# Routing by a running sum, the last product of layer 1 in two halves, and a later weight load in a three-stage kernel

## The chip, the cores and the metric

The kernel runs on one core of a Trainium2 chip. Its time is the device time of one execution in microseconds (us). Here it is a chain of dependent stages with one stream of instructions for each engine: TensorE (PE, with its weight loads as PEld), VectorE (DVE), ScalarE (ACT), GpSimd (POOL) and SyncE (SP, which here only issues DMAs). The streams meet through semaphores: an instruction waits until a semaphore has reached a value, and raises one when it is done.

## What is computed

Three layers follow each other: an attention with the queries pooled in pairs, a mixture of experts with a capacity (layer 1), and a second mixture of experts with a skip test and a residual (layer 2). All is float32. There are 2 x 8 heads over 1152 keys and 576 pooled queries, hence 1152 tokens of width 512; 8 experts with a hidden width of 1024.

```python
# attention (B=2, H=8, S=1152, D=64), pooled queries
q_pool = q.reshape(B, H, S // 2, 2, D).mean(axis=3)
scores = scale * np.matmul(q_pool, k.transpose(0, 1, 3, 2))
attn = softmax(scores)                 # sum + 1e-9
x = (attn @ v) -> [1152 tokens, 512]

# layer 1: a token goes to its best expert if that has room (capacity 288)
logits = x @ w_gate
expert_idx = np.argmax(logits, axis=1)
for i in range(N):                     # in the order of tokens
    if counts[e] < capacity:
        pos[i] = counts[e]; counts[e] += 1; keep[i] = True
h = relu(disp @ w1[e]); y = h @ w2[e]
out[i] = gate_w[i] * y                 # 0 where not kept

# layer 2: only tokens with x @ w_skip > 0
logits = xc @ w_gate2; e_idx = argmax(logits)
y[mask] = gate_w[mask] * (relu(xc[mask] @ w1[e]) @ w2[e])
out[do_compute] = xc + y               # else out = x
```

## The kernel before, in words

**Attention.** One head after the other. TensorE makes scores, turns the exponentials over with transposes, multiplies them by V and turns the result back (`turn_back`, L768, of the output tile `OT` that VectorE copies from the matmul buffers in `copy_output`, L1194). VectorE divides by the sums (`output_logits`, `output_x`), SP stores each head's 64 columns in DRAM (`store_x`, L436, four DMAs a head) and the logits of the routing come out of the same product, added over heads by `add_logits` (L1240) and `add_last_logits`.

**Routing** runs twice, as `for m in range(2)` on every engine (L855 on TensorE, L1362 on VectorE): m = 0 for layer 1, over 9 tiles of 128 tokens, and m = 1 for layer 2, over 14 tiles of 128 slots. VectorE finds each token's expert (`r_hot`, one column in eight is 1). TensorE counts with matmuls by triangular and full matrices of ones (L871 to L882) how many tokens of the same expert stand ahead of each one, and the total of each expert. These counts are in PSUM when `pos_ready` is raised. VectorE then makes of the totals how many grains of 64 rows each expert takes (`r_cmp`, `r_nt`), where each expert's grains begin (`r_sq`, `r_base`), adds that to the counts (`r_pos`), and cuts the slot into a tile number and a row in the tile (`r_which`, `r_inside`; L1404 to L1434). From these come `r_tile` and, three tiles at a time, `r_place`; POOL multiplies `r_tile` by token numbers (L655), and TensorE adds up in L890 which token stands in which slot. VectorE turns that into the list `rows_in` (L1443), and POOL fetches the first 128 rows from DRAM with an indirect DMA (`load_x`, L606) into `xraw`. Meanwhile VectorE prepares the gates (`r_gcut`, `r_ids`), TensorE sorts them (L898), and VectorE writes the tables of tiles and experts (`tab_n`, `tab_done`, `tab_grain`; `tables_ready` after L1464). Nearly every one of these VectorE instructions waits for the one before through a semaphore (`link`, L1328).

**Fillers.** Where TensorE would idle, it runs products of the identity with itself whose result nobody reads (`keep_busy`, L835, and the shorter `keep_briefly`). Their number is written into the program: 11 before the counting, 18 (m = 0) or 19 (m = 1) behind it, 16 or 12 behind the sorting of the gates. TensorE works its stream off in order, so what stands behind fillers starts only when they are through. The profile shows two records for each filler.

**Experts.** A tile of 128 rows is two grains of 64, which may belong to two experts. Weights lie in rings of four matrices (`w1ring`) and three (`w2ring`), loaded by SP in 4 pieces (`load_matrix`, L385). The upper grain's matrix is copied into `wright` by VectorE or ScalarE (`fill_right`, L323). A step on TensorE is `hidden_product(t)`, `y_product(t - 1)`, `turn_x(t + 1)`, `turn_hidden(t)`. Layer 1 has 10 tiles with these inputs and layer 2 has 9; the loops are written for the largest number, and an `If` in the body leaves the unused rounds empty. In layer 1, VectorE also makes the logits of layer 2 for each finished tile (`next_logits`, L1350: 9 multiply-and-add passes over `ysb`), after copying it. For the last tile this isn't done by VectorE: ScalarE copies the product (`ylast`, L1163), TensorE turns it (`turn_y`), ScalarE copies that (`yT`), TensorE multiplies by the weights of the logits, and ScalarE copies the nine columns into `logits2` (L1167). VectorE waits for that with `lg_copied`, for a value that it loads from the table `tab_n` (L1386), then starts the routing of layer 2.

**SP's order around the end of attention** is: store the last head (four DMAs, L458), wait until all is stored, load the first `w2` matrix of layer 1 (L464), wait until the first tile's rows have arrived, load the second `w2` matrix, and so on up to `wnext`, the weights for `next_logits`.

## Time and profile before

| | |
|---|---|
| median of 3 runs | 618.69 us (618.34 to 618.9) |
| the profiled execution | 618.62 us, of which the span of the profile is 616.9 us |
| granted TensorE clock, mean over the span | 0.995 of full speed |
| PE busy | 594.9 us, 96% of the span |
| DVE, ACT, POOL busy | 315.1, 266.9, 191.5 us |
| chain of waits | PE 90%, DMA 2%, DVE 2%, ACT 2%, "issue" 2% |

The chain of waits is followed back from the last instruction, at each step to what released it. TensorE's busy time holds the fillers too, so a busy TensorE isn't always one that does work. The three layers meet at two places: from about 270 to 291 us (attention to layer 1) and from about 446 to 467 us (layer 1 to layer 2). "Span" is what the trace covers; the time of the execution is 1.7 us more.

### The profile page before, as it was taken

The numbers are of one execution on the slowest core, as the hardware profiler recorded it, in microseconds if no ns is written. First come the engines' busy times: TensorE is split into PE (matmuls) and PEld (weight loads), VectorE is DVE, ScalarE is ACT, GpSimd is POOL, SyncE is SP. The second block draws the span as 40 slices with busy tenths as digits, with TensorE's granted clock in tenths as the row PEclk, the third lists the DMA queues.
The fourth block names the chain that finished last, engine by engine and source line by source line (L and its number), as shares of the span: only waits on it lengthen the run. The fifth ranks groups of instructions, "written<-read, shape, count | busy, mean of one in ns | idle before, by whom it ended". The sixth has DMA issues, their size and how long they took to land.

```text
span 616.9 us, 12447 instructions
## 1 busy us (share of the span) xinstructions
PE 594.9 (96%) x3719; PEld 352.3 (57%) x3720; DVE 315.1 (51%) x666; ACT 266.9 (43%) x439; POOL 191.5 (31%) x168
## 2 busy tenths in 40 slices
PE   8899999999999999998999999999999999999993
PEld 7677787877777777777333333333395333333331
DVE  5457565657575756656355652965574220322220
ACT  4655565655565656520244444444102444444410
POOL 4785635344453800001012221122211122222222
PEclk9999999999999999999999999999999999999997
DMA  8979818171721062006999397780846798841111
GB/s 201 291 184 258 186 39 173 39 166 45 153 50 26 11 232 87 22 9 208 399 391 409 124 352 275 284 307 29 305 174 229 274 312 322 321 150 43 45 52 61
DMA packets 42637, 111.61 MB, mean 181 GB/s; under 512 B 16020, under 2 KB 16020, under 8 KB 41536
## 3 DMA queue, kind: packets, MB, share of 16 engines
q1 hardware_dynamic: 38528, 99.03, 50.5%
q0 software_dynamic: 4080, 12.22, 5.7%
q8 instruction: 15, 0.25, 0.2%
q14 instruction: 14, 0.11, 0.1%
HBM read 102.68 MB, written 12.06 MB: 186 GB/s over the span
## 4 chain that ended last, share of the span: by engine, by line
PE 90%; DMA 2%; DVE 2%; issue 2%; ACT 2%; POOLq 0%; POOL 0%; SPq 0%; DVEq 0%; ACTq 0%
PE psum L929 41%; PE psum L704 14%; PE psum L718 11%; PE psum L752 9%; PE psum L916 4%; PE psum L838 3%; PE psum L780 3%; PE psum L764 1%; PE psum L748 1%; DMA xraw<-moe_in,rows_in 1%; DVE probs L1181 1%; ACT probs L1019 1%; PE psum L931 1%; DMA qraw<-in_q_dram 1%; DMA res<-moe_in,idx_r 1%
## 5 line engine op out<-in xcount | busy, mean ns | idle before, releaser
L929 PE MATMUL psum<-w1ring,XT 128*64 x304 | 134.5, 595 | 0.8 <-ACT XT L1126 0.4
L929 PE MATMUL psum<-w2ring,HT 128*64 x304 | 133.7, 592 | 1.7 <-DVE wright L323 1.7
L931 PE MATMUL psum<-wright,XT 128*64 128x512 f32 x304 | 134.5, 595 | 0.0
L931 PE MATMUL psum<-wright,HT 128*64 128x512 f32 x304 | 133.7, 592 | 0.0
L1181 DVE TENSOR_SCALAR_CACHE_REDUCE probs<-psum 128x1152 f32<-128x1152 f32 x72 | 97.5, 1357 | 62.6 <-PE psum L704 62.6
L1019 ACT ACTIVATE probs<-probs,nmax 128x1152 f32<-128x1152 f32 x72 | 90.7, 1260 | 45.6 <-DVE probs L1181 45.6
L704 PE MATMUL psum<-KT,QT 128*128 128x384 f32 x480 | 102.0, 350 | 3.0 <-DVE probs L1181 1.7
L929 PEld LDWEIGHTS psum<-w2ring,HT 128*64 128x64 f32 x304 | 41.5, 137 | 87.3 <-issue 87.3
L704 PEld LDWEIGHTS psum<-KT,QT 128*128 128x128 f32 x480 | 80.2, 188 | 15.0 <-issue 7.9
L929 PEld LDWEIGHTS psum<-w1ring,XT 128*64 128x64 f32 x304 | 40.1, 137 | 79.8 <-issue 79.8
L718 PE MATMUL psum<-ident,probs 128*128 128x128 f32 x648 | 82.0, 275 | 1.1 <-ACT probs L1019 0.6
L718 PEld LDWEIGHTS psum<-ident,probs 128*128 128x128 f32 x648 | 72.7, 140 | 9.2 <-issue 3.7
L1133 ACT ACTIVATE hid<-psum,slot_gate 128x1024 f32<-128x1024 f32 x19 | 21.2, 1114 | 125.2 <-PE psum L931 125.2
L1026 ACT COPY PT<-psum 128x512 f32<-128x512 f32 x88 | 48.4, 588 | 60.3 <-PE psum L718 60.3
L752 PE MATMUL psum<-PT,V 128*64 128x512 f32 x256 | 62.2, 605 | 0.0
L323 ACT COPY wright<-w1ring 128x1024 f32 x60 | 58.1, 1040 | 0.0
L323 DVE COPY wright<-w2ring 128x1024 f32 x76 | 49.1, 700 | 14.3 <-DMA w2ring<-in_moe_w_dram 14.2
L1348 DVE TENSOR_TENSOR orow<-psum,res 128x512 f32<-128x512 f32 x9 | 6.2, 691 | 97.0 <-PE psum L931 88.1
L1355 DVE CUSTOM_DVE_ANT_0 psum<-ysb,wnext 128x512 f32<-128x512 f32 x81 | 52.9, 723 | 0.0
L595 POOL COPY idx_x<-rows_in 128x1 int32 x15 | 8.8, 585 | 142.0 <-PE psum L916 142.0
L335 POOL CAST KT<-kraw 128x2304 fp32r<-128x2304 f32 x7 | 14.7, 2106 | 87.3 <-PE psum L704 82.8
L931 PEld LDWEIGHTS psum<-wright,HT 128*64 128x64 f32 x304 | 41.5, 137 | 0.0
(169 smaller groups left out, 645.7 us busy)
## 6 DMA issues: line engine op xcount, KB each, us to landing
w1ring<-in_moe_w_dram SPq DMA_DIRECT2D x64, 512.0 KB, 6.9
w2ring<-in_moe_w_dram SPq DMA_DIRECT2D x64, 512.0 KB, 7.1
qraw<-in_q_dram SPq DMA_DIRECT2D x30, 288.0 KB, 10.0
kraw<-in_k_dram SPq DMA_DIRECT2D x14, 576.0 KB, 9.2
V<-in_v_dram SPq DMA_DIRECT2D x8, 576.0 KB, 4.0
moe_in<-zero SPq DMA_DIRECT2D x9, 256.0 KB, 3.1
wnext<-in_next_w_dram SPq DMA_DIRECT2D x1, 2304.0 KB, 17.1
out_dram<-moe_in SPq DMA_DIRECT2D x1, 2304.0 KB, 9.4
```

Source lines behind the costliest of these rows:

```text
L323: copy(wright[k][:, part * PIECE:(part + 1) * PIECE], piece_of(k, slot, part).rearrange("p o f -> p (o f)")).then_inc(filled, 1)
L704: mm = pe.matmul(dst, QT[par][:, piece, q0:q0 + P], KT[par][:, b * S + c * KB:b * S + (c + 1) * KB], start=(i == 0), stop=(i == 2 * len(pa ...
L718: mm = pe.transpose(bank(T_BANK + place % 3)[:, i * P:(i + 1) * P], src, ident[:])
L752: mm = pe.matmul(psum[rows, PV_BANK, :], V[par][:, b * KT_N + j, :], PT[:, j, :], start=(j < 2), stop=False, skip_group_check=True)
L916: return pe.matmul(place[:, chunk * P:(chunk + 1) * P], src, ident[:], is_transpose=True, start=first, stop=False, skip_group_check=True)
L929: pe.matmul(psum[0:GRAIN, b, :], lhs[:, c * P:c * P + GRAIN], left, start=first, stop=last, skip_group_check=True)
L931: return pe.matmul(psum[GRAIN:P, b, :], lhs[:, c * P + GRAIN:(c + 1) * P], wright[k][:, cols], start=first, stop=last, skip_group_check=True)
L1019: nc.scalar.activation(probs[:, t, :], probs[:, t, :], ACT.Exp, bias=nmax[:, t:t + 1], scale=-1.0, accum_out=den[:, t:t + 1]).then_inc(pro ...
L1026: nc.scalar.copy(dst, bank(T_BANK + place % 3, cols)).then_inc(turned_by_act, 1)
L1133: nc.scalar.activation(hid[:].rearrange("p (c f) -> p c f", c=2), psum[:, HID_BANK:HID_BANK + 2, :], ACT.Relu, scale=g).then_inc(relu_read ...
L1181: nc.vector.tensor_scalar(probs[:, t, :].rearrange("p (c k) -> p c k", c=3), scores_in(h, t), -SCALE, None, ALU.mult, ALU.min, accum_out=n ...
L1355: nc.vector.tensor_tensor_reduce(out=bank(JUNK_BANK + e % 2), in0=ysb[:], in1=wnext[:, e, :], scale=1.0, scalar=0.0, op0=ALU.mult, op1=ALU ...
```

## The change

Six things are changed.

1. **Running sum (VectorE, both routings).** The totals are clamped (`r_held`), and one scan over 8 elements makes of them the running sum of rounded grains (`ends`). Adding a large number (`ROUND`) makes each partial sum round to a multiple of 64; a matmul of `whole` by `half_grain` adds the half grain that this needs. That replaces comparing, summing, multiplying by `earlier` and summing; and later, for the tables, multiplying by `upto` and summing. Some steps are joined into `scalar_tensor_tensor`, and some waits between neighbours fall away, since a semaphore of their own is waited for later.
2. **Fillers.** 14 instead of 18 and 19 behind the counting, 8 instead of 16 and 12 behind the sorting of the gates.
3. **SP.** The first `w2` matrix of layer 1 is loaded only when the first tile's rows have arrived. Of the last head's four stores, three no longer wait for the second batch's rows.
4. **The end of attention.** The last `OT` is copied in two halves of 256 columns, and `add_logits` goes ahead of that copy.
5. **The last product of layer 1** (`last_y_product`) is made in two halves of 256 columns into two banks. ScalarE copies the first while the second is made. The turned tile (`yT`) and the nine logits are now copied by VectorE.
6. **Gates of layer 1** are finished (`sum_gates`) before `rows_in` instead of behind it.

```diff
@@ SP
-            store_x(H - 1)
+            last_rows = token_rows(x_dram[0])
+            for i, written in ((0, 2 * H - 1), (1, 2 * H - 1), (3, 2 * H - 1), (2, 2 * H)):
+                sp.wait_ge(x_written, written)
+                parts, tiles, rows = last_rows[i]
+                sp.dma_start(rows[:, :, (H - 1) * D:H * D], xpair[parts, tiles, :]).then_inc(x_stored, 16)
             attention_over(sp)
             sp.wait_ge(zeroed, NT * 16)
             sp.wait_ge(x_stored, 16 * 4 * H)
+            sp.wait_ge(x_loaded_[0], 16)
             load_matrix(SECOND, 0, 0)
-            sp.wait_ge(x_loaded_[0], 16)
             load_matrix(SECOND, 0, 1)
@@ TensorE
                 pe.matmul(place_of(0, n), before[:], hot, start=True, stop=False, skip_group_check=True)
+                pe.matmul(place_of(n, n + 1), whole[:], half_grain[:].unsqueeze(1), start=False, stop=False, skip_group_check=True)
...
-                keep_busy((18, 19)[m], HID_BANK + 1)
+                keep_busy((14, 14)[m], HID_BANK + 1)
...
-                keep_busy((16, 12)[m], HID_BANK + 1)
+                keep_busy((8, 8)[m], HID_BANK + 1)
...
+                def last_y_product(t):
...
+                    for half in range(2):
+                        for c in range(FC):
...
+                            at = c * DM + half * 2 * P
+                            mm = product(SECOND, HT, (Y_BANK, X_BANK)[half], c, slice(at, at + 2 * P), slot,
+                                         c == 0, c == FC - 1, 2 * P)
+                        mm.then_inc((y_half, y_done)[half], 1)
@@ ScalarE
+                    act.wait_ge(y_half, 1)
+                    nc.scalar.copy(ylast[:, 0:2 * P], bank(Y_BANK, 2 * P)).then_inc(ylast_copied, 1)
                     act.wait_ge(y_done_[0], rest + (2 + START))
-                    nc.scalar.copy(ylast[:], bank(Y_BANK)).then_inc(y_copied_[0], 1)
-                    act.wait_ge(y_turned, 1)
-                    nc.scalar.copy(yT[:], bank(YT_BANK)).then_inc(yt_ready, 1)
-                    act.wait_ge(lg_done, 1)
-                    nc.scalar.copy(logits2[:, bass.ds(rest + 1, 1), :].rearrange("p o c -> p (o c)"), bank(LG_BANK, E + 1)
-                                   ).then_inc(lg_copied, 1)
+                    nc.scalar.copy(ylast[:, 2 * P:4 * P], bank(X_BANK, 2 * P)).then_inc(ylast_copied, 1)
@@ VectorE
+                link(nc.vector.tensor_scalar(r_held[:], tot, float(cap if m == 0 else B * SQ) + half, 1.0 + half, ALU.min, ALU.max))
+                link(nc.vector.tensor_tensor_scan(ends[:, 1:E + 1], r_held[:], r_held[:], ROUND + P, ALU.add, ALU.max))
...
                 with dve.Fori(1, NSLOT - 1) as t:
                     with dve.If(t < rest + 1):
                         step(t)
-                if m == 1:
+                if m == 0:
+                    for i in range(2):
+                        half = slice(i * 2 * P, (i + 1) * 2 * P)
+                        dve.wait_ge(y_turned, i + 1)
+                        nc.vector.tensor_copy(yT[:, half], bank(YT_BANK + i)[:, half]).then_inc(yt_ready, 1)
+                    at = bass.ds(rest + 1, 1)
+                    dve.wait_ge(lg_done, 1)
+                    nc.vector.tensor_copy(logits2[:, at, :].rearrange("p o c -> p (o c)"), bank(LG_BANK, E + 1)
+                                          ).then_inc(lg_copied, 1)
+                else:
                     copy_y(m, rest + 1)
```

VectorE's stream in the routing of layer 1, from the counts to `r_tile`, before:

```order
L1335 TENSOR_TENSOR r_cmp<-psum,grain_steps 128x8x5 [waits pos_ready]
L1338 TENSOR_REDUCE r_nt<-r_cmp 128x8 [waits route_step]
L1335 TENSOR_TENSOR r_sq<-r_nt,earlier 128x64 [waits route_step]
L1338 TENSOR_REDUCE r_base<-r_sq 128x8 [waits route_step]
L1420 TENSOR_SCALAR r_over<-psum 128x72 [waits route_step]
L1335 TENSOR_TENSOR r_pos<-psum,r_base 128x72 [waits route_step]
L1335 TENSOR_TENSOR r_pos<-r_pos,r_over 128x72 [waits route_step]
L1335 TENSOR_TENSOR r_pos<-r_pos,r_hot 128x72 [waits route_step]
L1338 TENSOR_REDUCE r_whole<-r_pos 128x9 [waits route_step]
L1431 TENSOR_SCALAR r_inside<-r_whole 128x9 [waits route_step]
L1432 TENSOR_SCALAR r_which<-r_whole 128x9 [waits route_step]
L1433 TENSOR_TENSOR r_tile<-iota_slot,r_which 128x126 [waits route_step]
```

The same stretch of VectorE's stream in the changed kernel (the row on `ends` is the scan):

```order
L1438 TENSOR_SCALAR r_held<-psum 128x8 [waits pos_ready]
L1439 SCALAR_TENSOR_TENSOR ends<-r_held 128x8 [waits route_step]
L1445 SCALAR_TENSOR_TENSOR r_kept<-psum,r_hot 128x72 [waits route_step]
L1446 SCALAR_TENSOR_TENSOR r_pos<-ends,psum 128x72
L1363 TENSOR_TENSOR r_pos<-r_pos,r_kept 128x72 [waits kept_ready,route_step]
L1366 TENSOR_REDUCE r_whole<-r_pos 128x9 [waits route_step]
L1452 TENSOR_SCALAR r_inside<-r_whole 128x9 [waits route_step]
L1453 TENSOR_SCALAR r_which<-r_whole 128x9
L1454 TENSOR_TENSOR r_tile<-iota_slot,r_which 128x126 [waits route_step]
```

Eleven instructions stood ahead of `r_tile`, each behind a wait for its neighbour; now there are eight, and two of them have no wait.

VectorE's stream from the last tile's logits in the loop of layer 1 to the start of the second routing, before:

```order
L1358 REGISTER_ALU
L1360 ISA [waits lrow_ready]
L1360 COPY logits<-lrow 128x9
L1497 UNCONDITIONAL_BRANCH
L1496 REGISTER_ALU
L1496 COMPARE_AND_BRANCH
L1386 TENSOR_LOAD tab_n
L1386 ISA x2
L1386 REGISTER_ALU
L1387 TENSOR_SCALAR active<-logits 128x14 [waits lg_copied]
```

And in the changed kernel:

```order
L1388 ISA [waits lrow_ready]
L1388 COPY logits<-lrow 128x9
L1518 UNCONDITIONAL_BRANCH
L1517 REGISTER_ALU
L1517 COMPARE_AND_BRANCH
L1524 COPY yT<-psum 128x256 [waits y_turned] x2
L1527 ISA [waits lg_done]
L1527 COPY logits<-psum 128x9
L1414 TENSOR_LOAD tab_n
L1414 ISA x2
L1414 REGISTER_ALU
L1415 TENSOR_SCALAR active<-logits 128x14 [waits lg_copied]
```

Three copies now stand between the end of the loop and the load of `tab_n`, and that load stands behind the copy of the last logits.

SP's stream at the end of attention, before and then changed; `moe_in<-xpair` are the stores of the last head, and the first `w2ring` row is the first `w2` matrix of layer 1:

```order
L441 DMA moe_in<-xpair 128x4x64 [waits x_written]
L441 DMA moe_in<-xpair 64x64
L441 DMA moe_in<-xpair 128x4x64
L441 DMA moe_in<-xpair 64x64
L397 DMA w2ring<-in_moe_w_dram 128x1024 [waits zeroed,x_stored,kq_cut,turned_back,logit_step]
L397 DMA w2ring<-in_moe_w_dram 128x1024 x3
L397 DMA w2ring<-in_moe_w_dram 128x1024 [waits x_loaded_0,w2_loaded_0]
```

```order
L457 DMA moe_in<-xpair 128x4x64 [waits x_written]
L457 DMA moe_in<-xpair 64x64 [waits x_written] x2
L457 DMA moe_in<-xpair 128x4x64 [waits x_written]
L392 DMA w2ring<-in_moe_w_dram 128x1024 [waits x_stored,zeroed,x_loaded_0,kq_cut,turned_back,logit_step]
L392 DMA w2ring<-in_moe_w_dram 128x1024 x3
L392 DMA w2ring<-in_moe_w_dram 128x1024 [waits w2_loaded_0]
```

The wait for `x_loaded_0`, the first tile's rows, has moved ahead of the first matrix.

## Rows read from the trace of the kernel before

**Rows 1.** The page, chain that ended last: share of the span by engine.
```profile
PE 90%; DMA 2%; DVE 2%; issue 2%; ACT 2%; POOLq 0%; POOL 0%; SPq 0%; DVEq 0%; ACTq 0%
```

**Rows 2.** Chain of waits, attention to layer 1: start us, us, what.
```profile
271.13 0.46 PE psum L748 x4
...
271.61 0.70 DVE OT L1200
...
276.41 4.12 PE psum L838 x36
...
281.85 0.18 DVE rows_in L1443
...
283.05 6.28 DMA xraw<-moe_in,rows_in
...
290.93 0.64 PE psum L929
```

**Rows 3.** Timeline, first routing: start us, us, engine, line, what [idle before <-releaser].
```profile
276.45 0.20 DVE L1335 TENSOR_TENSOR r_cmp<-psum,grain_steps 128x40 f32<-128x40 f32 x1 [0.51 <-PE psum L867]
...
279.17 0.29 DVE L1433 TENSOR_TENSOR r_tile<-iota_slot,r_which 128x126 f32<-128x126 f32 x1
...
279.64 0.55 POOL L655 TENSOR_TENSOR r_ids<-r_tile,token_id 128x126 fp32r<-128x126 f32 x1 [63.78 <-DVE r_tile L1433]
...
287.20 2.50 DVE L323 COPY wright<-w1ring 128x1024 f32 x4 [1.37 <-issue]
```

**Rows 4.** Timeline of SP's DMA issues at the end of attention.
```profile
280.61 10.58 SPq L397 DMA_DIRECT2D w2ring<-in_moe_w_dram  x8
```

**Rows 5.** Stretches: us, PE, PEld, DVE, ACT, POOL busy, PEclk, DMA share, GB/s.
```profile
286.00:287.00 1.00, 1.00 (x12) 1.00 (x11) 0.00 (x0) 0.00 (x0) 0.00 (x0) 1.00 0.96 340
462.00:463.00 1.00, 1.00 (x11) 1.00 (x11) 0.90 (x4) 0.00 (x0) 0.00 (x0) 1.00 0.44 139
```

**Rows 6.** Line L606 (fetch of rows), second routing, 455 to 470 us.
```profile
DMA to landing us min/median/max: 3.5/5.3/7.2
```

**Rows 7.** Timeline, end of layer 1.
```profile
446.59 0.17 DVE L1360 COPY logits<-lrow 128x9 f32 x1
...
447.26 0.66 PE L975 MATMUL psum<-ident,ylast 128*128 128x128 f32 x4
...
447.95 0.59 ACT L1165 COPY yT<-psum 128x512 f32<-128x512 f32 x1 [0.75 <-PE psum L975]
...
448.59 1.06 PE L982 MATMUL psum<-wcat,yT 128*128 128x9 f32 x8 [0.23 <-ACT yT L1165]
```

**Rows 8.** Chain of waits, end of the kernel: POOL's sequencer in empty rounds of its loop.
```profile
602.76 0.05 POOLq L671
...
604.05 0.05 POOLq L671
```

**Rows 9.** Timeline of VectorE: the one step of layer 1 that starts late on its side.
```profile
393.43 0.69 DVE L1345 COPY ysb<-psum 128x512 f32<-128x512 f32 x1 [1.25 <-issue]
```

**Rows 10.** Timeline, second routing.
```profile
449.98 0.17 DVE L1387 TENSOR_SCALAR active<-logits 128x14 f32<-128x14 f32 x1 [3.21 <-ACT logits L1167]
...
453.09 0.31 DVE L1335 TENSOR_TENSOR r_cmp<-psum,grain_steps 128x144 f32<-128x144 f32 x1
...
455.83 0.36 DVE L1433 TENSOR_TENSOR r_tile<-iota_slot,r_which 128x196 f32<-128x196 f32 x1
...
459.55 0.17 DVE L1443 TENSOR_SCALAR rows_in<-psum 128x14 int32<-128x14 f32 x1 [0.81 <-PE psum L890]
```

**Rows 11.** Chain of waits, second routing.
```profile
462.46 2.77 PE psum L838 x24
465.24 0.45 PE psum L916 x4
```

**Rows 12.** Stretches after TensorE's last product (columns as in rows 5).
```profile
607.00:608.00 1.00, 0.07 (x2) 0.00 (x0) 0.00 (x0) 0.00 (x0) 0.30 (x2) 1.00 0.35 49
...
610.00:611.00 1.00, 0.00 (x0) 0.00 (x0) 0.44 (x1) 0.00 (x0) 0.00 (x0) 0.84 0.00 0
```

More of the change, by code:

```diff
@@ L1425, in _ @@
-                if m == 0:
-                    with nc.allow_low_precision(reason="whole numbers far below 2 ** 24"):
-                        reduce(of(r_whole), of(r_pos), ALU.add)
-                else:
-                    reduce(of(r_slot), of(r_pos), ALU.add)
-                    tt(of(r_whole), of(r_slot), r_drop[:], ALU.add)
-                link(nc.vector.tensor_scalar(of(r_inside), of(r_whole), P - 1, None, ALU.bitwise_and))
+                    dve.wait_ge(kept_ready, 1)
+                tt(of(r_pos), of(r_pos), of(kept), ALU.mult)
@@ L1432, in _ @@
+                with nc.allow_low_precision(reason="whole numbers far below 2 ** 24"):
+                    reduce(of(r_whole), of(r_pos), ALU.add)
+                nc.vector.tensor_scalar(of(r_inside), of(r_whole), P - 1, None, ALU.bitwise_and).then_inc(inside_ready, 1)
                 link(nc.vector.tensor_scalar(of(r_which), of(r_whole), 7, None, ALU.logical_shift_right))
```

152 lines of the change are left out of this document (81 added, 71 removed).

## The prediction, made before the changed kernel had run

> **What bounds the kernel now.** I read the chain of waits by engine first: TensorE holds 90% of it, all else is a few per cent [rows 1]. The steps through experts are paced by TensorE's products, and the change leaves these as they are, except the last one of layer 1. So only the two crossings between layers can move the time. The chain, followed in order of time through them, is the second view. In the first crossing it runs through the copy of the output tile, the turning back, fillers, counting, fillers, the search for the rows, and then one long piece: 6.28 us of the DMA that fetches the first rows, before the first product starts at 290.93 [rows 2]. In the second it goes through ScalarE's copies between TensorE's small products [rows 7], VectorE's routing [rows 10], and the fillers in front of the first turning [rows 11]. The timelines of VectorE and SP, the third view, tell who is near behind the chain.
>
> **The sum** is made against the profiled execution, 618.62 us (span 616.9); the median of the runs is 0.07 above it.
>
> *First crossing, output tile and counting.* The full copy takes 0.70 [rows 2]. A copy of half the columns lies between 0.35 and 0.70; I take 0.42, since a copy has a fixed part. The turning back can then start 0.28 earlier, and its second half waits for nothing. The fillers behind it are unchanged in number and shift along; the added small counting matmul costs about 0.03. `add_logits`, moved ahead of the copy, runs while VectorE waits for TensorE's last product with V. **-0.25** (bounds 0 and -0.35).
>
> *First routing.* From `r_cmp` at 276.45 to `r_tile` at 279.17 [rows 3] eleven linked instructions take 2.72, so 0.247 each. Now there are eight, two of them without a wait, for which I take 0.14: 6 x 0.247 + 0.28 = 1.76, a gain of 0.96. The scan is shown by no row; over 8 elements I take it as one of the others, with bounds 0.17 and 0.6. `r_tile` is then 0.96 + 0.25 = 1.2 earlier, POOL's product, started at 279.64 and 0.55 long, ends at 279.0, and TensorE can add up the rows. It must first be through with the fillers: 36 records took 4.12 [rows 2], so 0.229 each filler of two records, four fewer are 0.92, and with the 0.25 they end 1.17 earlier. Both are ready 1.1 to 1.2 earlier than before, so `rows_in` moves from 281.85 [rows 2] to about 280.75. `sum_gates` now stands ahead of it, but ends at about 280.7 while VectorE would wait for TensorE anyway; if that cover is gone it costs up to 0.7. Beyond the 0.25: **-0.85** (bounds -0.2 and -1.0).
>
> *The first fetch.* In the kernel before, SP began to issue the first `w2` matrix at 280.61 [rows 4], 2.4 us ahead of the fetch, and while the fetch ran the DMA engines moved 340 GB/s at a share of 0.96 [rows 5]. The same fetch in the second routing has no matrix beside it (139 GB/s, share 0.44, [rows 5]) and lands in 3.5 us, against 7.2 for the one that follows it among weights [rows 6]. Holding the matrix back until the rows are there should give 3.5 in place of 6.28: **-2.78** (bounds 0 and -2.8). The last head's stores must have landed: only one of four is still issued behind the last rows, before the counts are in, and it has over 4 us until `rows_in`. What is late next? VectorE's copy of the first weights started at 287.20 [rows 3]. It stands behind the tables, which lose the 1.1, the 0.7 of `sum_gates` and two linked instructions (0.5): it starts at 284.9, and its first of four pieces is there at 285.5, before the product at 290.93 - 3.88 = 287.05. TensorE has eight fillers less (1.83) and is free at about 284.8, so it idles 0.7 until the rows land at 285.5. The fetch stays the bound. The first `w2` matrix, now issued at 285.6, needs about 5 us and is wanted after the first hidden product and the copy of the second tile's weights, near 297. Everything behind it on SP moves back about 2 us: the second and third matrices, and `wnext`. I count this as hidden, since the steps through experts are paced by TensorE.
>
> *End of layer 1.* In the kernel before, turning, ScalarE's copy and the product for the logits follow each other and end at 448.59 + 1.06 = 449.65 [rows 7]. With halves that overlap, this alone would end at about 448.9. But the copies of `yT` have gone to VectorE, and there they stand behind the loop over tiles. Its last logits end at 446.59 + 0.17 = 446.76 [rows 7]. The loop has 12 rounds, of which 8 are used: four empty rounds follow. POOL shows what such rounds cost: three in 604.05 - 602.76 = 1.29, so 0.43 each [rows 8]. VectorE is then free at 446.76 + 1.72 = 448.5, where its first half could have begun at about 447.4 (turning from 447.26). Two copies of 0.42, 0.35 apart, end at 449.3; TensorE's second half of the logits ends at 450.0, VectorE has copied the nine columns at 450.2. Then comes the second thing: the load of `tab_n` into a register stood in VectorE's idle time of 3.21 us before [rows 10] and now stands behind that copy. Its price is in rows 9: 1.25 us of idle time for one loop round, such a load and a few register instructions; less 0.43 it is 0.82. `active` starts at about 451.05 instead of 449.98. The Trainium skill puts the floor of a `tensor_load` at about 600 ns (DMA: Bandwidth & Descriptors, Latency and other measured facts); by it alone the sum would be 0.2 us lower, and the row agrees as far as it holds more than the load.
>
> The last product in halves has twice the instructions. The only products of 256 columns in the trace took 0.46 for 4 records [rows 2], so the 64 records of both halves would take up to 7.4 us, about 0.5 more than exact halves, or nothing more where that end is only modelled; I take 0.15. Together **+1.2** (bounds -0.7, if VectorE is free in time and the load hidden, and +2).
>
> *Second routing.* Before the counts, one instruction is shorter, one wait and `r_drop` are gone: VectorE comes 0.4 sooner to the counts. TensorE's counting then nearly binds, so -0.35. From `r_cmp` at 453.09 to `r_tile` at 455.83 [rows 10] ten linked instructions took 2.74. Seven remain, one without a wait, two on 8 elements only: 1.74, so -1.0. Five fillers less (1.14) let TensorE keep up. **-1.35**, `rows_in` then stands 0.15 earlier than before in all. From there two paths lead to the turning of the first rows, which was at 465.24 behind 24 records of fillers, 2.77 us [rows 11]. Four fillers less are -0.92. The fetch starts about 1.0 after `rows_in`, as in the first crossing (283.05 - 281.85 - 0.18, [rows 2]); `rows_in` ends at 459.55 + 0.17 [rows 10] - 0.15, so it starts at 460.5 and lands by 464.1, level with the fillers (464.2). I take **-0.85** (bounds 0 and -0.92).
>
> -0.25 - 0.85 - 2.78 + 1.2 - 1.35 - 0.85 = -4.9. From 618.62 that is 613.7, and with the 0.07 to the median 613.8.
>
> **Rivals.**
>
> *The halved end costs nothing.* For it: four empty rounds on VectorE might be faster than POOL's, and a load might be fetched while the last copy waits. Against it: the same three kinds of instruction make up a round on both engines, and VectorE's own row of 1.25 us [rows 9] fits POOL's. The stage would then stand as before or better, +1.2 gone: 618.7 - 6.1 = 612.6. Beside this, the Trainium skill gives 51 ns for a branch and 108 ns for a compare-and-branch (Advanced Engine Details and Errata, Control Flow Timing): a round of one and two of these would be 0.27 us, against the row's 0.43, and the sum would be 0.65 lower, halfway to this rival.
>
> *The first fetch isn't faster.* It is the first indirect DMA of the program, and if 6.28 us is its own start and not the matrix beside it, the 2.78 are not earned: 616.6. Against it: its landing at 289.3 comes just as the four pieces of the matrix are through.
>
> *Weights come too late.* The matrices after the first, and the second tile's fetch in between, are set back by some 2 us against a TensorE that is 3.9 us ahead. That second fetch took as long as one product lasts (7.2 in rows 6, between products of about 7), so each us more is paid in full. With 1 to 3 us given back: about 615.8.
>
> *Slower.* The fillers keep TensorE busy at the full clock (granted 1.00, 2.4 GHz), and twelve are gone at the first crossing, nine at the second. In the one place where I see the clock fall, the last product had ended at 607.07, the stretch from 607 was at 1.00, and it went to the lower level (1.2 GHz) within the stretch from 610 [rows 12], some 3.6 us after the product. If the first fetch still takes 6.28, TensorE idles from 284.8 to 288.3, 3.5 us, as long as there; then the first hidden product of about 7 us runs at the lower level, up to +7, which with the unearned 2.78 ends at up to 623.7. It decides from a fetch of over 6 us on; with 3.5 us the idle time is 0.7.
>
> **How the numbers follow.** Forecast 0.52 (613.8), halved end free 0.18 (612.6), fetch as slow as ever 0.13 (616.6), weights late 0.12 (615.8), slower 0.05 (620 to 624). The range of 8 in 10 reaches from 612.4, where the end costs nothing, to 616.6, and leaves out the clock and a part of the fetch. What a measurement can tell is about 0.2%, 1.2 us: faster than 617.5 holds in the forecast and nearly all of the next three, 0.92; within it 0.04; slower 0.04.
>
> **What would show it.** `DMA xraw` in the first crossing at 3.5 to 4 us; the first product at 287; VectorE's first copy of `yT` at about 448.5 less the shift, more than 1 us after the first half of the turning, and `active` 0.7 to 0.9 behind the end of the nine logits' copy; the span between the last product of layer 1 and `active` longer by 1 us or so than before; the `r_tile` rows about 1 us nearer to the counts; the clock at 1.00 throughout. It is wrong if the fetch still takes over 5 us, if TensorE waits for weights or rows in the first two tiles, or if `yT` is copied at once when it is turned.

## The result, and the profile after

| | before | changed |
|---|---|---|
| median | 618.69 us (618.34 to 618.9, 5 runs) | 615.66 us (614.51 to 616.29, 5 runs) |
| the profiled execution | 618.62 us, span 616.9 | 616.29 us, span 614.5 |
| granted TensorE clock over the span | 0.995 | 0.992 |

The ratio is 0.995 (95% interval 0.9939 to 0.9961): 3 us faster, in the predicted range (612.4 to 616.6), and 1.9 us slower than the forecast of 613.8. The profiled execution is the slowest of the five; its clock in the second crossing and its tail, below, account for part of that. TensorE's share of the chain (page, as in [rows 1]) has fallen from 90% to 88%:

```profile
PE 88%; DVE 3%; issue 3%; DMA 2%; ACT 2%; POOLq 0%; DVEq 0%; POOL 0%; SPq 0%; ACTq 0%
```

**First crossing.** The chain of waits, attention to layer 1 (start us, us, what; compare [rows 2]):

```profile
271.55 0.43 DVE OT L1224
...
276.11 3.23 PE psum L840 x28
...
280.66 0.18 DVE rows_in L1467
...
281.87 3.68 DMA xraw<-moe_in,rows_in
...
285.59 0.67 PE psum L919 x4
...
287.14 0.64 PE psum L932
```

VectorE's timeline of the same stretch (start, us, engine, line, what, [idle before <-releaser]; compare [rows 3]):

```profile
276.14 0.17 DVE L1438 TENSOR_SCALAR r_held<-psum 128x8 f32<-128x8 f32 x1 [0.54 <-PE psum L869]
276.34 0.18 DVE L1439 TENSOR_TENSOR_SCAN ends<-r_held 128x8 f32<-128x8 f32 x1
...
277.77 0.29 DVE L1454 TENSOR_TENSOR r_tile<-iota_slot,r_which 128x126 f32<-128x126 f32 x1
...
284.67 2.50 DVE L318 COPY wright<-w1ring 128x1024 f32 x4 [1.38 <-issue]
```

And SP's issues (compare [rows 4]):

```profile
285.70 5.58 SPq L392 DMA_DIRECT2D w2ring<-in_moe_w_dram  x6
```

The matrix is issued at 285.70, behind the landing of the rows, and the fetch takes 3.68 in place of 6.28. `rows_in` is 1.19 earlier, the first product 290.93 - 287.14 = 3.79 earlier. This lead stays through layer 1: a turning late in it stands in the chain at 418.26, before at 422.02, 3.76 apart. No weight is late.

**End of layer 1.** The chain (compare [rows 7]; DVEq is VectorE's sequencer, and line 1518 is the `If` in a round of its loop, so it shows once in each of the four empty rounds):

```profile
443.24 0.07 DVEq L1518
...
443.82 0.06 DVEq L1518
...
444.36 0.06 DVEq L1518
...
444.90 0.06 DVEq L1518
...
445.26 0.44 DVE yT L1524
...
446.80 4.14 PE psum L840 x22
```

Four empty rounds, (444.90 - 443.24) / 3 = 0.55 each, stand between the last tile's logits and the copy of `yT`. The timelines of the three engines that take part, and VectorE's on to `rows_in` (compare [rows 7, 10]):

```profile
443.33 0.60 PE L998 MATMUL psum<-ident,ylast 128*128 128x128 f32 x4
...
445.26 0.76 DVE L1524 COPY yT<-psum 128x256 f32<-128x256 f32 x2 [2.25 <-issue]
...
445.74 1.06 PE L1006 MATMUL psum<-wcat,yT 128*128 128x9 f32 x8 [1.36 <-DVE yT L1524]
...
446.98 0.17 DVE L1527 COPY logits<-psum 128x9 f32 x1 [0.97 <-PE psum L1006]
...
447.74 0.17 DVE L1415 TENSOR_SCALAR active<-logits 128x14 f32<-128x14 f32 x1 [0.59 <-DVE logits L1527]
...
451.60 0.17 DVE L1438 TENSOR_SCALAR r_held<-psum 128x8 f32<-128x8 f32 x1 [1.07 <-PE psum L869]
...
453.22 0.36 DVE L1454 TENSOR_TENSOR r_tile<-iota_slot,r_which 128x196 f32<-128x196 f32 x1
...
456.94 0.17 DVE L1467 TENSOR_SCALAR rows_in<-psum 128x14 int32<-128x14 f32 x1 [0.81 <-PE psum L893]
...
461.86 0.42 PEld L919 LDWEIGHTS psum<-ident,xraw 128*128 128x128 f32 x4 [0.31 <-DMA xraw<-moe_in,rows_in]
```

The last row is the first turning of layer 2. Before, the same row read:

```profile
464.96 0.47 PEld L916 LDWEIGHTS psum<-ident,xraw 128*128 128x128 f32 x4
```

At the end of layer 1 the first half of the last tile's turning was there from about 443.6, and its copy starts at 445.26: TensorE stands idle for 1.36. `active` is only 449.98 - 447.74 = 2.24 earlier than before, so 3.76 - 2.24 = 1.5 us of the lead is gone here. What follows was not predicted. TensorE's clock, in stretches of one microsecond (us, PE, PEld, DVE, ACT, POOL busy, PEclk, DMA share, GB/s):

```profile
444.00:445.00 1.00, 0.38 (x4) 0.19 (x2) 0.00 (x0) 0.00 (x0) 0.33 (x1) 1.00 0.00 0
445.00:446.00 1.00, 0.26 (x3) 0.26 (x3) 0.74 (x2) 0.00 (x0) 0.67 (x1) 1.00 0.00 0
446.00:447.00 1.00, 1.00 (x11) 1.00 (x11) 0.03 (x2) 0.00 (x0) 0.00 (x0) 1.00 0.60 230
447.00:448.00 1.00, 1.00 (x10) 1.00 (x9) 0.41 (x3) 0.00 (x0) 0.00 (x0) 0.74 0.00 0
448.00:449.00 1.00, 1.00 (x6) 1.00 (x6) 0.90 (x5) 0.30 (x1) 0.00 (x0) 0.50 1.71 590
...
450.00:451.00 1.00, 1.00 (x10) 0.94 (x10) 0.47 (x3) 0.00 (x0) 0.00 (x0) 0.55 0.15 49
```

It falls to the lower level (1.2 GHz, 0.50) while TensorE is fully busy with the 11 fillers ahead of the counting. Two thinly used microseconds (444 to 446) and a fully busy one at 1.00 (446 to 447) came before it. The 11 fillers, 22 records, take 4.14, where 22 at the full clock take 2.50 (in the chain of the first crossing, from 273.20), and VectorE waits 1.07 for the counts that stand behind them. The lead shrinks from 2.24 at `active` to 453.09 - 451.60 = 1.49 at the counts.

**Tail.** The chain at the end of the kernel, with the last fetch of the residual:

```profile
594.32 0.60 PE psum L919 x4
...
602.94 4.42 DMA res<-moe_in,idx_r
```

That fetch took 3.68 before, so another 0.7 goes here: the last turning is 597.52 - 594.32 = 3.20 earlier, the end of the span 2.4.

### The profile page after: what moved, and what is told of

Read it like the earlier page. It is cut to its first block, busy times and chain, and to the rows that moved or that the text cites. A ratio compares the mean times of both kernels' runs of the same rounds, so it can differ in the third digit from the quotient of the medians.

```text
span 614.5 us, 12427 instructions
## 1 busy us (share of the span) xinstructions
PE 591.7 (96%) x3711; PEld 351.9 (57%) x3712; DVE 313.5 (51%) x659; ACT 266.3 (43%) x438; POOL 188.5 (31%) x164
## 4 chain that ended last, share of the span: by engine, by line
PE 88%; DVE 3%; issue 3%; DMA 2%; ACT 2%; POOLq 0%; DVEq 0%; POOL 0%; SPq 0%; ACTq 0%
PE psum L932 40%; PE psum L701 14%; PE psum L715 12%; PE psum L749 9%; PE psum L919 4%; PE psum L782 3%; PE psum L840 2%; PE psum L761 1%; PE psum L745 1%; DVE probs L1204 1%; ACT probs L1045 1%; PE psum L934 1%; DMA qraw<-in_q_dram 1%; DMA res<-moe_in,idx_r 1%; DMA xraw<-moe_in,rows_in 1%
## 5 line engine op out<-in xcount | busy, mean ns | idle before, releaser
L934 PE MATMUL psum<-wright,HT 128*64 128x512 f32 (+1 forms) x320 | 133.7, 571 | 0.0
L932 PEld LDWEIGHTS psum<-w2ring,HT 128*64 128x64 f32 x320 | 43.7, 137 | 85.0 <-issue 83.0
L934 PEld LDWEIGHTS psum<-wright,HT 128*64 128x64 f32 x320 | 43.7, 137 | 0.0
```

Source lines behind the costliest of these rows:

```text
L932: pe.matmul(psum[0:GRAIN, b, 0:width], lhs[:, c * P:c * P + GRAIN], left, start=first, stop=last, skip_group_check=True)
L934: return pe.matmul(psum[GRAIN:P, b, 0:width], lhs[:, c * P + GRAIN:(c + 1) * P], wright[k][:, cols], start=first, stop=last, skip_group_ch ...
```

## The experiments

Every kernel was timed beside the kernel before, whose median was 618.43 beside e1 to e4, 618.57 beside e5 to e8, 618.87 beside e9 to e11 and 618.54 beside e12. So medians of different groups can differ by 0.4 for no reason in the kernels; where the text compares across groups, the traces decide. No run takes the new order of the stores, the half copy at the end of attention or the earlier `sum_gates` alone. Line numbers differ a little from kernel to kernel; names don't.

**e1, the copies back on ScalarE.**

```diff
@@ ScalarE, after the copy of ylast
+                    for i in range(2):
+                        act.wait_ge(y_turned, i + 1)
+                        nc.scalar.copy(yT[:, half], bank(YT_BANK + i)[:, half]).then_inc(yt_ready, 1)
+                    act.wait_ge(lg_done, 1)
+                    nc.scalar.copy(logits2[...], bank(LG_BANK, E + 1)).then_inc(lg_copied, 1)
@@ VectorE, behind the loop over tiles: the same three copies taken out
```

> The changed kernel, with one thing undone: the two half copies of yT and the copy of the nine logits are made by ScalarE again; the product stays in halves. Delay theory (VectorE comes out of four empty loop rounds too late, the load of tab_n stands behind its copy, and TensorE idling there lets its clock fall): from the end of the last product of layer 1 to `active` takes about 2.7 us less than 4.9 of the change's profile brought it to, hence about 3.0; no stretch under 1.00 in the clock; `active` to the counts about 2.8 instead of 3.9; time about 613.0, that is 2.7 below the change's 615.7. Rival (the clock falls for another reason, such as the small products of this stretch): the copies gain 1.5, but a stretch at 0.5 stays and the counts come late; about 614.3. Rival (ScalarE's copies are as slow as VectorE's wait): within 0.3 of 615.7.

Measured: 612.27 (612.16 to 612.56), ratio 0.990 (0.9885 to 0.9915); 3.4 us faster than the changed kernel.

```profile
443.71 0.65 ACT L1195 COPY yT<-psum 128x256 f32<-128x256 f32 x2 [0.48 <-PE psum L998]
...
445.32 0.17 ACT L1197 COPY logits<-psum 128x9 f32 x1 [0.97 <-PE psum L1006]
...
445.99 0.17 DVE L1422 TENSOR_SCALAR active<-logits 128x14 f32<-128x14 f32 x1 [2.98 <-ACT logits L1197]
```

`active` is 1.75 earlier than in the changed kernel. It still starts 0.5 after the logits are there (445.32 + 0.17 = 445.49): VectorE's empty rounds and its load of `tab_n` end only then, as e8 and e10 show, where both are gone. The clock stays at 1.00 through the crossing. The place of the three copies is the cause of the loss, not the halving. Of the 3.4 us, 1.75 is there at `active`. In the two profiled executions the fallen clock and the longer last fetch of the changed kernel make up most of the rest, 1.0 from `active` to the counts (3.86 against 2.83) and 0.8 in the fetch (4.42 against 3.60). Neither belongs to every execution of the changed kernel (e12, e11).

**e2, the end of layer 1 as before.** The whole `last_y_product`, the halves of `turn_y` and both `ylast` copies undone, on top of e1.

```diff
-                if m == 1:
-                    y_product(rest + 1)
-                else:
-                    last_y_product(rest + 1)
+                y_product(rest + 1)
```

> The changed kernel with the whole end of layer 1 as in the kernel before: product in one piece of 512 columns, ylast, yT and the nine logits copied by ScalarE in one piece each. It tells what the halving itself is worth beside the copies that went to VectorE. Theory: halves overlap and end about 0.6 us earlier, so this kernel is 0.6 above the one with ScalarE's half copies, about 613.6. Rival: the halves gain nothing (256-column products cost what the overlap gives): level with it, 613.0. Both say that it is faster than the change, by some 2 us, if the delay theory holds.

Measured: 612.69 (612.64 to 613.27), 0.9911 (0.9895 to 0.9926). `active` starts at 445.97, as in e1 (445.99), since VectorE is not free before, and the counts (448.82) and `rows_in` (454.16 and 454.15) stand alike too. The two profiled executions, 612.66 and 612.56, are 0.1 apart. So with the copies in the right place the halving gains nothing up to `rows_in`; the 0.4 between the medians is too small to be put down to it. The product itself, from its first record to the fillers behind it, takes 7.02 whole and 7.06 in halves (e1).

**e3, eight fillers in front of the product for the logits.**

```diff
-                    keep_busy(2, HID_BANK + 1)
+                    keep_busy(8, HID_BANK + 1)
```

> The changed kernel with 8 instead of 2 fillers between the turning of the last tile and the product for the logits, which covers most of the 1.4 us in which TensorE waited for VectorE's copy of yT. Theory (the idle time lets the clock fall, and the fall costs 0.8 to 1.1 us): clock at 1.00 through the crossing, 11 fillers in 2.5 instead of 4.1 us, time about 614.8, and the spread of the runs narrower. Rival (the clock falls whatever TensorE does there): the same 615.7 with a stretch at 0.5. The delay itself stays: `active` no earlier.

Measured: 614.55 (614.38 to 615.5), 0.9941 (0.9927 to 0.9954); 1.1 below the changed kernel. The copies are as late as ever (VectorE idles 2.25 ahead of them, as in the changed kernel; they start at 445.00, there at 445.26, with the whole stream 0.2 to 0.3 earlier), but the clock, through the stretches where it was 0.74 and 0.50, reads:

```profile
447.00:448.00 1.00, 1.00 (x11) 1.00 (x11) 0.48 (x3) 0.00 (x0) 0.00 (x0) 1.00 0.73 246
448.00:449.00 1.00, 1.00 (x10) 0.91 (x9) 0.88 (x4) 0.30 (x1) 0.00 (x0) 1.00 1.40 492
```

From `active` to the counts it is 450.46 - 447.49 = 2.97, in place of 451.60 - 447.74 = 3.86. The clock's fall is a cost by itself, of about 0.9, beside that of the late copies. That the fillers prevented it is not shown by one profile: without them it failed to come in e11 and e12 too. All five executions of e3 have a mean clock of 0.994 or 0.995, which fits.

**e4, VectorE's loop in groups of four rounds**, copies left on VectorE: an empty group is skipped as a whole.

```diff
-                with dve.Fori(1, NSLOT - 1) as t:
-                    with dve.If(t < rest + 1):
-                        step(t)
+                with dve.Fori(0, (NSLOT - 2) // GROUP) as g:
+                    with dve.If(g * GROUP < rest):
+                        with dve.Fori(0, GROUP) as i:
+                            t = dve.snap(g * GROUP + (i + 1))
+                            with dve.If(t < rest + 1):
+                                step(t)
```

> The changed kernel with VectorE's loop over tiles written as TensorE's is: groups of four rounds with an If around each group, so that one empty outer round is left in layer 1 instead of four empty rounds. Theory: the empty rounds cost about 0.55 us each on VectorE, so it is free about 1.6 us earlier, yT is copied when it is turned, TensorE idles under 0.5 us, no fall of the clock; the load of tab_n (0.6 us) stays. Time about 613.6. Rival (the wait before yT is not the rounds but another cost of leaving the loop): 615.7, with the same gap of about 2.3 us between the last logits of the loop and yT.

Measured: 612.72 (612.61 to 613.0), 0.9907 (0.9892 to 0.9923).

```profile
443.90 0.76 DVE L1527 COPY yT<-psum 128x256 f32<-128x256 f32 x2 [0.76 <-PE psum L998]
```

VectorE now waits for TensorE, not for its loop. With the copies where the change put them, taking the empty rounds away gives 2.9 us, 1.2 of it at `active` (446.54), and the clock stays at 1.00: the rounds, and in the profiled execution of the changed kernel the clock behind them, are the loss. The load of `tab_n` is left (idle time of 0.75 in front of `active`).

**e5, the kernel before, with the first `w2` matrix held back and nothing else.**

```diff
             sp.wait_ge(x_stored, 16 * 4 * H)
-            load_matrix(SECOND, 0, 0)
             sp.wait_ge(x_loaded_[0], 16)
+            load_matrix(SECOND, 0, 0)
```

> The kernel before with one thing changed: SP waits for the first tile's rows ahead of the first w2 matrix of layer 1. Theory (the matrix beside it made the first fetch slow, and behind the fetch the fillers are next): the fetch takes about 3.7 instead of 6.28 us and lands at 286.7, but the 16 fillers keep TensorE until 288.3, so only 0.9 us of the 2.6 is earned: time 617.5. Rival (the first indirect DMA of the program is slow by itself): fetch 6.3, time 618.4. Rival (the later matrices are missed): fetch 3.7 and TensorE waits for weights or rows in the first tiles, time over 618.4.

Measured: 617.15 (616.88 to 617.34), 0.9978 (0.9968 to 0.9987). The first product of layer 1, in its chain:

```profile
289.67 0.64 PE psum L929
```

**e6, the same with 8 in place of 16 fillers** in front of the first turning (`keep_busy((8, 12)[m], HID_BANK + 1)`).

> As the one before, and 8 instead of 16 fillers behind the sorting of the gates in the first routing. Theory: TensorE is free at 286.5, the fetch lands at 286.7, the turning moves from 289.38 to 286.8, time 618.4 - 2.6 = 615.8. Rival (VectorE's copy of the first weights, which starts at 287.20, is next): its first piece is there at 287.9, and the product starts at about 288.3 all the same. Rival (a clock that falls for lack of fillers): a stretch under 1.00 at 286 to 290 and a time over 616.5.

Measured: 616.07 (615.74 to 616.16), 0.9957 (0.9944 to 0.997). The chain of e6:

```profile
283.25 3.66 DMA xraw<-moe_in,rows_in
...
288.54 0.64 PE psum L929
```

The fetch is fast by the held matrix alone, with neither the running sum nor the new stores in the kernel. It takes 3.66 in e6 and 3.8 in e5, against 6.28. Of this gain only 290.93 - 289.67 = 1.3 us reach the first product while TensorE still has 16 fillers to work off; with eight, 290.93 - 288.54 = 2.4 do. The medians agree, with 1.4 and 2.5 below the kernel before.

**e7, e1 with the matrix ahead of the rows again.**

```diff
             sp.wait_ge(x_stored, 16 * 4 * H)
-            sp.wait_ge(x_loaded_[0], 16)
             load_matrix(SECOND, 0, 0)
+            sp.wait_ge(x_loaded_[0], 16)
             load_matrix(SECOND, 0, 1)
```

> The changed kernel with ScalarE's half copies at the end of layer 1 (612.3 us), and the first w2 matrix loaded before the first rows as in the kernel before. Theory: the fetch takes 6.3 again, the first product starts 2.6 us later, time 614.9, and the clock stays at 1.00 although TensorE idles some 3.4 us ahead of the turning. Rival (the fall of the clock that the prediction took as its slower case): TensorE idles 3.4 us, the first hidden product of 7 us runs in part at 1.2 GHz, time 616 to 621. Rival (the store order or the shorter routing shortened the fetch): within 0.3 of 612.3.

Measured: 616.4 (614.1 to 617.58, six runs), 0.9961 (0.9946 to 0.9977): 4.1 above e1, where the longer fetch (6.59 against 3.65 in e1) accounts for 2.9. Its chain, and stretches of it:

```profile
281.84 6.59 DMA xraw<-moe_in,rows_in
...
288.47 0.80 PE psum L919 x4
...
290.55 1.05 PE psum L932
```

```profile
286.00:287.00 1.00, 0.00 (x0) 0.00 (x0) 1.00 (x2) 0.00 (x0) 0.00 (x0) 1.00 1.00 410
...
290.00:291.00 1.00, 1.00 (x5) 0.55 (x6) 0.00 (x0) 0.00 (x0) 0.82 (x1) 0.50 0.82 266
```

Both mechanisms of the prediction's rival "slower" are here: TensorE, short of fillers, idles 3.75 us, and then works at 0.50 until it recovers within the stretch from 292. In this execution that costs 1.3 us and not 7 (the turning of the first rows is 288.47 - 285.58 = 2.9 behind e1, the first turning of hidden rows 299.71 - 295.51 = 4.2), and the median is still below the kernel before. The price isn't the same in every execution: the fastest, at a mean clock of 0.996, took 614.1, and the slowest, at 0.988, took 617.58, so up to 3.5 us may go with the clock. Only the execution of 616.71 was profiled. The expectation that the clock would hold was wrong; its rival, 616 to 621, has the measured median.

**e8, all empty rounds away.** e1 with VectorE's loop as in e4, POOL's loop over tiles grouped in the same way, and the number of tiles kept in its register:

```diff
-                    dve.wait_ge(lg_copied, dve.value_load(tab_n[0][:], min_val=0, max_val=NSLOT - 2) + 2)
+                    dve.wait_ge(lg_copied, rest + 2)
```

> The changed kernel with ScalarE's half copies, VectorE's and POOL's loops over tiles in groups of four, and no second load of tab_n (the value that the loop of layer 1 used is kept in its register). Theory: `active` follows the copy of the nine logits at once, 0.45 earlier than in the kernel with ScalarE's copies alone, of which the 11 fillers let 0.3 through to the counts; at the end of the kernel POOL has two empty rounds in place of five, the last fetch of the residual starts 1.2 us earlier and lands still after the last product: time 612.3 - 1.5 = 610.8. Rival (the end of the kernel isn't set by POOL): 612.0.

Measured: **610.92** (610.8 to 611.16), 0.9877 (0.9862 to 0.9891): the fastest of all, 4.7 us below the changed kernel. `active` starts at 445.56, the last residual fetch at 598.35 (599.93 in e1).

**e9, e1 with the fillers of before.**

```diff
-                keep_busy((14, 14)[m], HID_BANK + 1)
+                keep_busy((18, 19)[m], HID_BANK + 1)
...
-                keep_busy((8, 8)[m], HID_BANK + 1)
+                keep_busy((16, 12)[m], HID_BANK + 1)
```

> The kernel of e1 (both yT halves and the nine logits copied by ScalarE, 612.27 us) with the numbers of fillers of the kernel before: 18 and 19 behind the counting in place of 14 and 14, 16 and 12 behind the sorting of the gates in place of 8 and 8. Theory (fillers bind, so that a shorter routing on VectorE earns only what TensorE's stream lets through): in the first crossing TensorE is through with its stream 12 x 0.229 = 2.7 us later than with the short numbers, of which about 0.7 was idle time, so the first turning comes about 2.0 later, near 287.5, waits for no DMA, and the first product near 289.1; in the second, nine more fillers are 2.06, of which some 1.5 are paid. Time 612.3 + 3.5 = 615.8. Rival (VectorE's linked instructions were the bound, the fillers only lay beside them): rows_in stays where it is in both crossings, at most the 12 and 8 fillers in front of the first turning are seen, 0.3 to 0.9 in each, and the time is 612.9 to 613.8.

Measured: 616.14 (615.77 to 616.6), 0.9957 (0.9943 to 0.9971): 3.9 above e1. In the chain of the first crossing the fillers now stand where the fetch did:

```profile
284.29 3.67 PE psum L840 x32
287.96 0.45 PE psum L919 x4
```

The fillers behind the counting hold `rows_in` up as well: the fetch starts at 283.29, in e1 at 281.89, and in the second crossing VectorE idles 1.90 ahead of `rows_in`, in e1 0.81. That refutes the rival. With the old number of fillers TensorE's stream, and no longer the rows, sets the first turning. So more than half of what the change gives with the copies on ScalarE is only there once the fillers are taken out; in e9, where all else is as in e1, 2.7 of 6.2 us are left.

**e10, e8 without POOL's grouping.**

> The kernel of e8 (610.92 us) with POOL's loop over tiles as in the changed kernel: only VectorE's loop is in groups of four, and the number of tiles is not loaded a second time from tab_n. Theory (POOL's empty rounds stand in the chain at the end of the kernel, 0.43 us each, five less a group's own round, and the last fetch of the residual starts that much later): active at 445.6 and the last turning at 590.8 as in e8, the last residual fetch starts at 599.4 in place of 598.35, time 610.9 + 1.1 = 612.0. Rival (the last fetch and its wait hide POOL's rounds, and e8's gain over e1 came from VectorE): 610.9 to 611.2.

Measured: 611.89 (611.56 to 611.98), 0.9887 (0.9872 to 0.9903). The last residual fetch starts at 599.32, not 598.35: POOL's empty rounds at the end of the kernel cost 1.0. VectorE's rounds and the load, with the copies on ScalarE, cost about 0.5 at `active` (445.43, in e1 445.99, with the stream ahead of it 0.1 earlier); the medians, 612.27 and 611.89, are 0.4 apart.

**e11, the changed kernel without the second load of `tab_n`** (the diff of e8's `wait_ge`, alone).

> The changed kernel in which VectorE waits for the last logits by the number of tiles that it already holds in a register, so that the load of tab_n behind the copy of the nine logits goes away; empty rounds and all else stay. Theory (the load costs about 0.6 us at active, but TensorE's 11 fillers in front of the counting then bind, since its clock has fallen to the lower level in them): active starts right behind the logits' copy, near 447.2 in place of 447.74, the fillers still take 4.1 us and end near 451.7, r_held at 451.5, and the time stays at 615.3 to 615.8. First rival (the load is free, the 0.59 us of idle time is the semaphore's or the engine's own): active stays at 447.7. Second rival (all of the 0.6 us reaches the end, the fillers do not bind): 615.0, with r_held at 451.0.

Measured: 613.79 (613.54 to 615.14), 0.9924 (0.991 to 0.9937): 1.9 below the changed kernel, and below every time named above. TensorE's and VectorE's timelines:

```profile
445.72 1.06 PE L1006 MATMUL psum<-wcat,yT 128*128 128x9 f32 x8 [1.40 <-DVE yT L1524]
446.63 2.70 PE L840 MATMUL psum<-ident 128*128 128x128 f32 x22
...
447.16 0.17 DVE L1415 TENSOR_SCALAR active<-logits 128x14 f32<-128x14 f32 x1
```

The load is worth the 0.58 by which `active` is earlier. But the clock did not fall either, though TensorE's stream up to there is the same and it idled for 1.40: the fillers took 2.70 from first start to last end, in this view 4.29 in the changed kernel. Four executions lie at 613.54 to 613.84 with a mean clock of 0.995 or 0.996, one at 615.14 with 0.993. What I had taken for a property of the changed kernel might be one of an execution.

**e12, the changed kernel once more, without an edit.**

> The changed kernel without an edit, once more. Five executions of it gave 614.51 us at a mean clock of 0.995 and 615.52 to 616.29 at 0.992 to 0.994; five of the kernel of e11 gave 613.54 to 613.84 at 0.995 and 0.996, and 615.14 at 0.993. Theory (the same program falls to the lower clock in the second crossing in some executions and not in others, at a price of 1.1 to 1.4 us, and the load of tab_n is worth a further 0.6): both levels show again, near 614.5 and near 615.7, the low ones at 0.995, most of them the higher time, and the median lies between 614.4 and 616. Rival (the fall belongs to the second load of tab_n, which e11 does without): all executions lie near 615.7 with a clock of 0.992 to 0.994.

Measured: 615.02 (614.43 to 616.12), 0.9947 (0.9933 to 0.996); in order 614.63, 616.12, 615.47, 614.43, 615.02 at mean clocks of 0.994, 0.992, 0.993, 0.995, 0.995. The profiled execution is the one of 614.63, and the same program as above reads:

```profile
448.00:449.00 1.00, 1.00 (x12) 1.00 (x10) 0.90 (x5) 0.30 (x1) 0.00 (x0) 1.00 2.08 737
```

```profile
445.65 1.06 PE L1006 MATMUL psum<-wcat,yT 128*128 128x9 f32 x8 [1.40 <-DVE yT L1524]
446.57 2.70 PE L840 MATMUL psum<-ident 128*128 128x128 f32 x22
449.85 0.22 PE L873 MATMUL psum<-r_hot,before 128*128 128x112 bf16 x1 [0.57 <-DVE r_hot L1427]
...
450.63 0.17 DVE L1438 TENSOR_SCALAR r_held<-psum 128x8 f32<-128x8 f32 x1 [0.18 <-PE psum L869]
```

Here the fillers do not bind, the counting waits for VectorE, and it starts at 449.85 in place of 450.73. With the same instructions and nearly the same idle time (1.40 and 1.36) the clock fell in one execution and not in another. From `active` to the counts this one takes 450.63 - 447.66 = 2.97, the other 3.86, so the fall cost 0.89. The two executions are 616.29 - 614.63 = 1.66 apart; the rest is 0.3 from `rows_in` to the turning (4.92 and 4.64), 0.3 in the last fetch (4.42 and 4.08) and 0.1 ahead of `active`. The rival, that the second load brings the fall, is refuted: the same program, load and all, gave both.

## Why the prediction was right, and where it was off

The direction held, and so did the mechanism of the likeliest case. Five of the six steps lie within their bounds, and the sixth had none. The forecast was 1.9 us too good, and in the profiled execution the largest single part of that is the clock in the second routing.

The time alone would have misled: 615.66 lies 0.1 from the 615.8 of the rival "weights come too late", which did not happen, and 1.9 from the forecast. That it fell into the range owes something to luck, since the range reached so far up for another reason, a fetch that stays slow.

*First crossing.* The half copy took 0.43 (0.42 assumed), the counts came 0.31 sooner (0.25), `rows_in` 1.19 sooner (1.10). The scan took 0.18, the low end of its bounds. The fetch took 3.68 (3.5), and 3.79 stood at the first product against 3.88. By e5 and e6 the fetch's gain is due to the held matrix, by e9 much of the crossing's gain needs the fillers taken out. TensorE idled 0.84 (0.7) ahead of the turning and nothing was late, as forecast.

*Later weights.* Hidden, as forecast: 3.79 at the first product, 3.76 at the turning late in layer 1. That rival is out.

*End of layer 1.* The mechanism was right (VectorE in empty rounds behind its last logits; then the load of `tab_n` behind the copy), its price 1.5 in place of 1.2. Two terms were off in opposite ways. The rounds were 0.55 each on VectorE, where I had 0.43 from POOL, so four cost 0.5 more. The load was 0.58 (e11 against the profile of the changed kernel), where I had 0.82. The Trainium skill gives a floor of about 600 ns for a `tensor_load` (DMA: Bandwidth & Descriptors, Latency and other measured facts), and the trace agrees. It gives 51 and 108 ns for branches (Advanced Engine Details and Errata, Control Flow Timing); the prediction's estimate of 0.27 from these is half of what a round took. For the product in halves I had allowed 0.15; e1 and e2 show 0.04.

*Second routing: the step that failed.* I had put -0.35 ahead of the counts and "the clock at 1.00 throughout", and had let the clock fall only after an idle time of over 3 us at the first crossing. In the profiled execution it fell after an idle time of 1.36 between two short groups of products, and the stretch from `active` to the counts cost 0.75 instead of gaining 0.35: an error of 1.1. The two profiles of one program (the changed kernel's and e12's) show that 0.89 of this is the clock's fall. It isn't a property of the change alone but of some executions of it; what decides between them no run shows. Where the clock stayed at 1.00, as in e1, the counts come 448.82 - 445.99 = 2.83 behind `active`, before 3.11 [rows 10]: -0.28, close to the -0.35.

*After the counts.* From the counts to `rows_in` -1.12, as assumed (-1.35 + 0.35 = -1.0). From there to the turning -0.49, not -0.85: the turning's first weight load moved by 3.10 (464.96 to 461.86) where `rows_in` had moved by 2.61, and TensorE waited 0.31 for a fetch that took 3.8. Fillers and fetch had been put level; the fetch was the later.

*The tail* was taken as unchanged. The last fetch took 4.42 in this execution, 4.08 in e12 and 4.04 in e3, but 3.60 to 3.68 in e1, e2, e4, e8 to e11 and before. That is 0.4 to 0.7, and what sets it no run shows; the copies on VectorE alone don't, since e4 and e11 have them too.

In the profiled execution: -3.79 (first crossing) + 1.55 (end of layer 1) + 0.75 (to the counts) - 1.12 - 0.49 (to the turning) - 0.1 (layer 2) + 0.8 (tail) = -2.4, against -2.33 measured. The mechanism of the likeliest case was right, and the rivals "end costs nothing" and "fetch as slow as ever" are refuted in this kernel by the rows above and by e1, e4, e5 and e7. The clock's fall was in no case of the prediction for this place. Where the rival "slower" put it, at the first crossing, e7 has it: the 7 us allowed for a whole product at the lower level were far too many (1.3 in the profiled execution, 3.5 between the fastest and the slowest).

## What to carry to other kernels

Work moved to an engine starts when that engine's own loop ends, empty rounds included: before moving a copy to a "free" engine, read what its sequencer does there, and group a loop's rounds or put the copy where the loop is done. Fillers, the arithmetic that they cover and the transfer behind them have to be shortened together; each alone gives a part (e5, e6, e9). When fillers are taken out or a copy comes late, price the gaps of TensorE at both levels of its clock, and profile more than one execution before a fall is taken for a property of the kernel. The mean clock over the span is only a rough sign of it: an execution of e1 with 0.993 took 612.25, another with 0.995 took 612.16.

## What the hardware showed that was not expected

- The granted clock fell to 0.50 for about three microseconds, amid fully busy fillers, after a gap of only 1.36 us between small products. In another profiled execution of the same program (e12) it did not. Of ten executions of the changed kernel the five with a mean clock of 0.992 or 0.993 took 615.47 to 616.29, the three with 0.995 took 614.43 to 615.02, and the two with 0.994 took 614.63 and 615.52. The Trainium skill says that the point at which the clock rises varies between runs of the same kernel (TensorE: Matmul & The Clock Gate, Part 1: The HAM clock gate). The two profiles here agree that executions differ, and go further: in one the clock did not fall in this place at all.
- An idle time of 3.75 us had the same kind of fall (e7), at a price of 1.3 us in the profiled execution; its six executions spread over 3.5 us.
- The first fetch of 128 rows took 3.7 to 3.8 us with the weight load held back, and 6.3 to 6.6 beside a weight load of the same moment.
- An empty round of a loop with an `If` cost 0.55 us on VectorE and 0.43 on POOL; a scan over 8 elements took 0.18.
